# Two chained layers behind packed attention: the first eight hidden sums as plain fp32 products, and M's parts made later

## What is computed

```
p_packed = softmax(p k^T / 8) v          # 8 batches, 8 heads, 32 packed rows, 576 keys, 64 dims
attn     = softmax(q p_packed^T / 8) p_packed   # 576 tokens a batch
x  = attn as (4608 tokens, 512)
x1 = (h - tanh(h)) @ w_out,  h = x @ w_in       # w_in 512 x 2048, w_out 2048 x 512
y  = (s * relu(h2)^2 + b) @ w_out2,  h2 = x1 @ w_in2
```

## Time and profile before

| | |
|---|---|
| runs | 1424.15, 1425.27, 1425.74 us, median 1425.27 |
| the profiled execution | 1425.8 us, its span 1424.0 us |
| TensorE busy | 1415.6 us, 99% |
| VectorE busy | 956.9 us, 67% |
| ScalarE busy | 699.1 us, 49% |
| GpSimd busy | 43.4 us, 3% |

### The profile page before, as it was taken

One profiled execution on the slowest core, in us unless ns is written; L12 is line 12 of the kernel. 1 busy time (PEld: TensorE's weight loads), 2 busy tenths in 40 slices (PEclk: granted clock), 3 DMA queues, 4 the chain that ended last, 5 costly groups with the idle time before them and its releaser, 6 DMA issues.

```text
span 1424.0 us, 23054 instructions
## 1 busy us (share of the span) xinstructions
PE 1415.6 (99%) x8414; PEld 1158.7 (81%) x8414; DVE 956.9 (67%) x1716; ACT 699.1 (49%) x1368; POOL 43.4 (3%) x38
## 2 busy tenths in 40 slices
PE   8999999999999999999999999999999999999999
PEld 6777878787878878888998888888888888888887
DVE  7897878787878778776576545755466454854553
ACT  5777666666666665754343223622245223722243
POOL 1120000000000000000000000000000000000000
PEclk9999999999999999999999999999999999999999
DMA  9789778787877766589696554764556644766135
GB/s 370 267 273 308 265 246 276 231 271 242 283 246 231 254 198 223 183 266 346 243 370 247 210 224 167 256 257 176 227 205 253 227 169 182 277 226 232 59 133 192
DMA packets 107775, 338.63 MB, mean 238 GB/s; under 512 B 26000, under 2 KB 37392, under 8 KB 97936
## 3 DMA queue, kind: packets, MB, share of 16 engines
q1 hardware_dynamic: 107520, 336.57, 66.8%
q10 hardware_dynamic: 144, 0.59, 0.1%
HBM read 282.59 MB, written 54.53 MB: 237 GB/s over the span
## 4 chain that ended last, share of the span: by engine, by line
PE 96%; DMA 2%; DVE 2%; ACT 0%; issue 0%; SPq 0%; DVEq 0%; ACTq 0%
PE banks L309 27%; PE banks L310 26%; PE banks L311 26%; PE banks L856 4%; PE banks L858 4%; PE banks L857 4%; PE banks L685 2%; PE banks L642 1%; DMA x_operands_wide_raw<-x1T_scratch 1%; PE banks L666 1%; DMA w_out_raw<-w_out 1%; PE banks L700 1%; PE banks L650 0%; DMA kT_first<-k_T 0%; PE banks L675 0%
## 5 line engine op out<-in xcount | busy, mean ns | idle before, releaser
L309 PE MATMUL banks<-g_high,w_out_ring 128*128 128x512 f32 x1152 | 458.4, 398 | 0.3 <-DVE g_low L1816 0.2
L310 PE MATMUL banks<-g_low,w_out_ring 128*128 128x512 f32 x1152 | 450.8, 391 | 0.0
L311 PE MATMUL banks<-g_high,w_out_ring 128*128 128x512 f32 x1152 | 449.0, 390 | 0.0
L309 PEld LDWEIGHTS banks<-g_high,w_out_ring 128*128 128x128 f32 x1152 | 216.1, 188 | 69.1 <-issue 30.8
L1323 ACT ACTIVATE g<-g,small 128x512 f32<-128x512 f32 x144 | 117.3, 815 | 295.6 <-DVE g L1812 294.9
L311 PEld LDWEIGHTS banks<-g_high,w_out_ring 128*128 128x128 f32 x1152 | 216.4, 188 | 47.5
L310 PEld LDWEIGHTS banks<-g_low,w_out_ring 128*128 128x128 f32 x1152 | 216.7, 188 | 34.9
L309 PE MATMUL banks<-x_operands_wide,w_in_first 128*128 128x512 f32 x448 | 174.3, 389 | 0.0
L310 PE MATMUL banks<-x_operands_wide,w_in_first 128*128 128x512 f32 x448 | 174.3, 389 | 0.0
L311 PE MATMUL banks<-x_operands_wide,w_in_first 128*128 128x512 f32 x448 | 174.3, 389 | 0.0
L1816 DVE TENSOR_TENSOR g_low<-g,g_high 128x512 fp32r<-128x512 f32 x144 | 99.0, 688 | 48.8 <-ACT g_high L1327 48.8
(11 more groups left out here) (192 smaller groups left out, 2076.3 us busy)
## 6 DMA issues: line engine op xcount, KB each, us to landing
w_out_ring<-w_out_parts_scratch SPq DMA_DIRECT2D x272, 512.0 KB, 4.3
w_in_first<-w_in_operands_scratch SPq DMA_DIRECT2D x28, 1792.0 KB, 7.2
w_in_ring<-w_in SPq DMA_DIRECT2D x32, 1024.0 KB, 8.0
qT<-q_T SPq DMA_DIRECT2D x16, 576.0 KB, 8.6
x1T_scratch<-out_store SPq DMA_DIRECT2D x9, 1024.0 KB, 5.8
v_rows<-v_rows SPq DMA_DIRECT2D x8, 1024.0 KB, 6.7
w_out_parts_scratch<-w_out_ring SPq DMA_DIRECT2D x16, 512.0 KB, 6.5
w_out_parts_scratch<-w_out_stage SPq DMA_DIRECT2D x16, 512.0 KB, 9.2
```

Of the source, the lines that this page charges most:

```text
L309: nc.tensor.matmul(out, high, rhigh, start=first, stop=False)
L310: nc.tensor.matmul(out, high, rlow, start=False, stop=False)
L311: return nc.tensor.matmul(out, low, rhigh, start=False, stop=last)
```

## The change

On TensorE the sums e = 0 to 7 become two plain fp32 products each (unsplit M in `MB_RAW[:, :, 4:6]`, unsplit probabilities in `AT_RAW[0]`), where they were six fp32r products. Both stretches of zero products are taken out. Sums 8 to 15 stay split and now wait for `m_first`, raised once for each pair of blocks.

On ScalarE `m_first_round` copies M unrounded to another place, in the same two copies a round; round 1 now stands right behind the exponentials. `high2_half` is gone. Four new copies `high_m(p)` make M's high parts between the tanhs. `high_w_out1(0)`, `(1)` move from behind `tanh_plain(3)` to behind `tanh_plain(8)`, `(2)` behind `(9)`, `(3)` behind `(11)`. `exp1(2)` and `exp1(3)` stood around `tanh_plain(10)`; now they stand behind `tanh_plain(10)` and, after `high_w_out1(3)`, behind `tanh_plain(11)`.

On VectorE the two low parts of the probabilities and all five M subtractions of before are gone; four new ones, `m_low(p)`, read both inputs from SBUF and stand behind `minus_plain(3)`, `(5)`, `(7)` and `(9)`. `max1(2)` and `max1(3)` move from ahead of `minus_plain(8)` to behind `m_low(3)` and behind `minus_plain(11)`.

```diff
+    def m_plain(p):
+        return MB_RAW[:, p, 4:6, :, :].rearrange("p x k f -> p (x k) f")
 # TensorE
             def plain(e):
-                if u == 0:
-                    pe.wait_ge(m_first, (1, 2, 3, 3, 4, 4, 5, 5)[f])
                 if e == 2:
                     pe.wait_ge(turn2_done, 1)
                 if e >= 4:
                     pe.wait_ge(g_done, e - 3)
+                if u == 0:
+                    pe.wait_ge(m_first_out, 2 * (f // PLAIN) + 2)
+                    for k in range(KM):
+                        if e == 0:
+                            pe.wait_ge(back2_first, k + 1)
+                        last = nc.tensor.matmul(out, MB_RAW[:, f // 2, 4 + x, k, :], AT_RAW[0][:, k, 1, :],
+                                                start=(k == 0), stop=(k == KM - 1))
+                else:
+                    pe.wait_ge(m_first, f // 2 + 1)
+                    pe.wait_ge(at_plain, 1)
...
             pe.wait_ge(turn2_first, 2)
-            warm(7, 5)
-            for e in range(4):
+            for e in range(7):
                 plain(e)
-            warm(5, 1)
-            plain(4)
-            plain(5)
-            plain(6)
             scores1(1, 0)
             plain(7)
             scores1(1, 1)
 # ScalarE
             def m_first_round(k):
                 act.wait_ge(m_done, k + 1)
                 for g in range(KM):
-                    nc.scalar.copy(MB[:, 2 * k:2 * k + 2, g:4:2, 0, :],
+                    nc.scalar.copy(MB_RAW[:, 2 * k:2 * k + 2, 4:6, g, :],
+            def high_m(p):
+                act.wait_ge(m_first_out, 2 * (p // 2) + 2)
+                nc.scalar.copy(MB[:, p, 0:4, 0, :], m_plain(p)).then_inc(m_first_high, 1)
...
             tanh_plain(2)
+            high_m(0)
             tanh_plain(3)
-            high_w_out1(0)
-            high_w_out1(1)
-            for e in range(4, 7):
-                tanh_plain(e)
+            high_m(1)
+            tanh_plain(4)
             high2_plain()
+            tanh_plain(5)
+            high_m(2)
+            tanh_plain(6)
+            high_m(3)
             tanh_plain(7)
             copy_s1(1, 0)
             copy_s1(1, 1)
+            tanh_plain(8)
+            high_w_out1(0)
+            high_w_out1(1)
+            tanh_plain(9)
             high_w_out1(2)
-            tanh_plain(8)
+            tanh_plain(10)
+            exp1(2)
+            tanh_plain(11)
             high_w_out1(3)
-            tanh_plain(9)
-            exp1(2)
-            tanh_plain(10)
             exp1(3)
-            tanh_plain(11)
             high_g1(0)
             high_g1(1)
 # VectorE
+            def m_low(p):
+                dve.wait_ge(m_first_high, p + 1)
+                nc.vector.tensor_tensor(MB[:, p, 0:4, 1, :], m_plain(p), read(MB[:, p, 0:4, 0, :]), ALU.subtract
                                         ).then_inc(m_first, 1)
...
             minus_plain(3)
+            m_low(0)
             low2_plain()
-            for e in range(4, 8):
-                minus_plain(e)
+            minus_plain(4)
+            minus_plain(5)
+            m_low(1)
+            minus_plain(6)
+            minus_plain(7)
+            m_low(2)
+            minus_plain(8)
+            minus_plain(9)
+            m_low(3)
             max1(2)
+            minus_plain(10)
+            minus_plain(11)
             max1(3)
-            for e in range(2 * PLAIN, 3 * PLAIN):
-                minus_plain(e)
             low_g1(0)
             low_g1(1)
```

More of the change, by code:

```diff
@@ L283, in build @@
     exp2_first, sum2_first, norm2_first = sem("exp2_first"), sem("sum2_first"), sem("norm2_first")
-    back2_first, high2_first, at_first = sem("back2_first"), sem("high2_first"), sem("at_first")
-    m_first, m_first_high = sem("m_first"), sem("m_first_high")
+    back2_first = sem("back2_first")
+    m_first_out, m_first_high, m_first = sem("m_first_out"), sem("m_first_high"), sem("m_first")
     at_plain_high, at_plain = sem("at_plain_high"), sem("at_plain")
@@ L713, in plain @@
                     pe.wait_ge(g_done, e - 3)
-                if e == 2 * PLAIN:
+                out, x = banks[:, plain_bank(e), 0:U1], f % 2
+                if u == 0:
[7 more added lines that the diff above has]
+                    pe.wait_ge(m_first, f // 2 + 1)
                     pe.wait_ge(at_plain, 1)
[L716 to L719, removed]
+                    m = lambda k, part: MB[:, f // 2, 2 * x + k, part, :]
+                    a = lambda k, part: AT[1][:, 2 + k, part, :]
                     for k in range(KM):
[L722 to L731, removed]
+                        last = product(out, m(k, 0), m(k, 1), a(k, 0), a(k, 1), k == 0, k == KM - 1)
                 last.then_inc(h_done, 1)
@@ L1012, in m_first_round @@
                 for g in range(KM):
-                    nc.scalar.copy(MB[:, 2 * k:2 * k + 2, g:4:2, 0, :],
+                    nc.scalar.copy(MB_RAW[:, 2 * k:2 * k + 2, 4:6, g, :],
                                    banks[:, m_banks(k) + g, :].rearrange("p (a x f) -> p a x f", a=2, x=2)
-                                   ).then_inc(m_first_high, 1)
+                                   ).then_inc(m_first_out, 1)
+            def high_m(p):
+                act.wait_ge(m_first_out, 2 * (p // 2) + 2)
+                nc.scalar.copy(MB[:, p, 0:4, 0, :], m_plain(p)).then_inc(m_first_high, 1)
             def m_round(k):
@@ L1038, in exp2_half @@
                 nc.scalar.activation(E2[:, 0, k, :], E2[:, 0, k, :], ACT.Exp, scale=SCALE).then_inc(exp2_first, 1)
-            def high2_half(k):
-                act.wait_ge(back2_first, k + 1)
-                nc.scalar.copy(AT[1][:, k, 0, :], AT_RAW[0][:, k, 1, :]).then_inc(high2_first, 1)
             def high2_plain():
@@ L1134, in _ @@
                 exp2_half(k)
-            for k in range(KM):
-                high2_half(k)
             m_first_round(1)
@@ L1480, in softmax2_first @@
                     nc.vector.tensor_tensor(rows(k), rows(k), spread(max2[0], k), ALU.subtract).then_inc(sub2_first, 1)
-                m_first_low(0)
                 for k in range(KM):
@@ L1494, in softmax2_first @@
                     nc.vector.transpose(AT_RAW[0][:, k, 1, :], E2[:, 0, k, :]).then_inc(back2_first, 1)
[L1495 to L1499, removed]
             def turn2(w):
@@ L1638, in _ @@
             turn2(1)
-            m_first_pair(1)
             def minus_plain(e):
@@ L1668, in _ @@
             sub2(1)
-            m_first_pair(2)
-            m_first_pair(3)
             minus_plain(0)
```

## The result

The changed kernel takes 1428.85 us (median of ten runs, 1427.56 to 1430.63) against 1425.19 us before (ten runs): **3.66 us slower**, a ratio of 1.0026 with a 95% interval of 1.0016 to 1.0036. The forecast was 1426.6, the clock rival 1428.9. The profiled execution took 1427.7 us, one of the fastest of the ten and 1.9 over the profiled one of before.

A forecast was written before the change was run, and what follows sets the result against it. TensorE, busy 99%, was taken to bound the kernel. The transpose behind sum 15 would start 1.14 us late, plus 0.12 for the port, taken as +1.3: 1427.1 us profiled, 1426.6 median; range 1424.9 to 1428.9.

The forecast's parts named there:

- the clock rival: TensorE idling 3.5 us ahead of the transpose drops the clock to 1.2 GHz: total +3.2 to +4.1, 1428.9 us; chance 13%.
- TensorE's terms: Sums 0 to 7 at 0.97 us each without zero products: sum 8 at 28.85 instead of 30.83, 2.0 us earlier.
- The weight loads: Rival: weight loads of the plain fp32 products don't hide, 3.5 us more ahead of sum 8: +4.7, 1430.0 us; chance 4%.
- The chain: From sum 8, ScalarE and VectorE wait for each other in turn: w_out's opening transpose at 39.70 instead of 38.56, 1.14 late.
- The port: m_low(3) meets GpSimd at the shared port: 0.12 us lost if VectorE is next; rival GpSimd next, 1.38, 1427.8 us, chance 17%.
- The sum: Transpose 1.26 us late with the port, nearly nothing given back later: +1.3 us, narrow ends +1.0 and +1.5.
- The price of the clock: Half-speed stretch of 3.8 us behind the hole loses 1.9 us, one half as long again 2.8.
- Is it given back?: At the score block at 51.62, 0.26 us might be regained; from pair 4 on no long wait takes up lateness.

The follow-up runs named there:

- e6: The kernel before with only the first maxima and exponentials of blocks 2 and 3 moved as in the change: 1427.92 against 1425.02 us, +2.90.
- e5: The changed kernel with both stretches of zero products put back: 1430.94 us against 1425.02 for the kernel before, +5.92 (four runs).
- e1: The changed kernel with max1(2) and max1(3) put back ahead of minus_plain(8): 1426.00 us against 1425.88 for the kernel before, +0.12.
- e10: The changed kernel timed again with no edit: 1428.18 us against 1425.38 for the kernel before, +2.80.
- e3: The changed kernel with high_w_out1(0) and (1) put back ahead of tanh_plain(4): 1426.57 us against 1425.88 for the kernel before, +0.69.
- e2: The changed kernel with the hole filled by thirteen zero products ahead of the transpose's wait: 1427.44 us against 1425.88 for the kernel before, +1.56.
- e7: The changed kernel with four zero products splitting the hole in two: 1426.76 us against 1425.02 for the kernel before, +1.74.
- e8: The changed kernel, maxima back, GpSimd's third and fourth w_out subtraction held until low_g1(1) is done: 1424.82 us against 1425.02 before, -0.20.

## Why the prediction was right and wrong

- **TensorE's terms: right.** A plain sum took 6.96/7 = 0.99 us against 0.97, sum 8 started at 28.83 against 28.85, the hole was 3.1 us against 3.5 (counted from the last product's end, it begins at 36.66, not at 36.2). The agreement of sum 8 to 0.02 us is in part luck: sum 0 started 0.22 us earlier than I had it, and the longer sums used that up. The weight loads hid.
- **The chain: right.** The transpose was forecast at 39.70, with the port at 39.82, and started at 39.75. e6 and e5 show the chain's cause and its start, e1 that it is the maxima.
- **The port: right on who is next,** since `m_low(3)` took 0.76 us. That the same port would take 1.0 us from `low_g1(0)` in e1, once the chain was mended, I hadn't worked out.
- **The sum: one term missing.** Lateness was put at 1.3 us and is 1.56 in the filled hole. The clock was put at nothing, with a chance of 13% for 1.9 to 2.8 us; it fell in 19 of 21 executions and costs 1.5 to 1.6 us in the traces, 1.2 to 2.1 in the medians. The failed step is the weighing of that rival: "dense work lies on both sides" is no protection. Its own sign of being wrong, products of 512 columns near 0.43 us apart behind the hole, is what the profile shows (0.42). The Trainium skill (TensorE: Matmul & The Clock Gate, "Why this matters for your kernels") warns of idle gaps between bursts; the change agrees with the warning, at 19 of 21, and it deserved the larger chance.
- **The price of the clock: somewhat high.** The 1.9 us came from the zero products at the start of the span, 0.236 us apart. PEclk reads 1.00 there too, so no row shows that they ran at the lower level that the change shows at 40 us.
- **The number: luck at the edge.** The measured 1428.85 lies 2.3 us over the forecast and 0.05 inside the range, which reached so far only because half of the clock rival had been taken in. On a time within 0.2% of before I had put 0.80, on a slower one 0.18; the first timing is 0.26% slower, the second 0.19%.
- **Is it given back?** I expected 0.26 us at most at the score block, and TensorE's lateness went from 2.77 us at 41.6 to 2.58 at 54, so yes, at that size. That nothing behind it could take up more was wrong by a little: 0.4 us more went at 73 us, where the kernel before waits ahead of a transpose. From there the lateness stood at 2.2 us up to 327 us, and the span ended 1.9 later.

## What to carry to other kernels

When a stream on the binding engine is shortened, follow the order of work on the engines that feed it up to the next wait: here a maximum and an exponential put behind a subtraction of the same round trip turned the gain into idle time. Price idle time on TensorE twice, once as lateness and once as the clock behind it. If a hole can't be avoided, fill it with products of zeros: that takes away the clock's part, not the lateness. When a chain is mended, look again at what now meets at VectorE's and GpSimd's shared port.

## What the runs showed of the hardware

- The clock fell in a share of executions that grew with the hole: none of 11 at 1.7 us, 2 of 10 at 2.1, 4 of 11 at 2.5, 19 of 21 at 3.1 (2 of 4 in e5), and 3 of 11 for 1.0 and 0.9 us with 0.9 us of zero products between. The kernel before, without a hole, lost it in 1 of 81. I had expected all or nothing. The kernels of this row differ in more than the hole and ran on several chips, so the growth is what these counts show and no rule.
- One fall costs about 1.5 us: from one group of transposes to the next it takes 4.86 us in the change, 4.96 in e10 and 4.81 in e3, against 3.35 at full clock behind a wait (e2, e5, e6, e7) and 3.28 without a wait (the kernel before). Seven executions show a mean of 0.998, which asks for more than 4 us at the lower level (an estimate from 1426 us of span); none of them was profiled.
- Beside GpSimd's subtractions two VectorE subtractions with both inputs in SBUF take 2.28 us (e1) and 2.38 (e8) instead of 1.29.
- Two kernels that differ only in the order of two stores and a load lose or keep 1.4 us at 92 us in their profiled executions with the same median: what such late loads hang on stays open.
